# Set-up and first tile of a fused convolution and two-layer MLP kernel on one core: put-off low parts, an earlier split, PE work during the convolution, paired remainders

## The reference, cut to what matters

```python
out = np.einsum('hk,bskhg->bshg', softmax(weight), x_unfolded)   # convolution
h = x @ w_in1;  g = h / (1 + exp(-1.702 h));  x2 = g @ w_out1    # layer 1
h = x2 @ w_in2
P = a0 + a1*h + a2*h**2 + a3*h**3
Q = 1 + |b0|*|h| + |b1|*h**2
out = (P / (Q + 1e-6)) @ w_out2                                  # layer 2
```

## Time and profile before

| | |
|---|---|
| Median of three runs | 1391.59 us (1391.28 to 1391.95) |
| The profiled execution: its own time | 1396.26 us |
| The profiled execution: span in the trace | 1394.1 us |
| PE busy | 1324.5 us, 95% of the span, 4800 instructions |
| DVE, ACT, POOL busy | 1107.4 (79%), 979.4 (70%), 326.0 (23%) us |
| First matmul of step n = 0 | 25.33 us into the span |
| DMA | 20.37 MB, 15 GB/s on the mean |

### The profile page before, as it was taken

The page is one execution under the profiler, slowest core; times in us unless marked ns, Lnnn a source line. Parts: engine busy times, 40 slices in busy tenths (PEclk is TensorE's granted clock), DMA queues, the critical chain, the costliest instruction groups (busy, mean ns, idle before and its releaser), DMA issues. The chain is left out here.

```text
span 1394.1 us, 14800 instructions
## 1 busy us (share of the span) xinstructions
PE 1324.5 (95%) x4800; PEld 699.2 (50%) x4800; DVE 1107.4 (79%) x1204; ACT 979.4 (70%) x1161; POOL 326.0 (23%) x150
## 2 busy tenths in 40 slices
PE   2999999999999999999999999999999999999876
PEld 1445555555555555555555555555555555545332
DVE  5228888888888888888888888888888888877885
ACT  4237767777776777777777777777777777776774
POOL 3202222222222222222222222222222222222222
PEclk9999999999999999999999999999999999999998
DMA  8100000000000000000000000000000000000000
GB/s 207 38 12 0 11 1 23 1 12 12 1 23 0 23 0 11 11 0 23 0 23 0 11 11 0 23 0 23 0 11 12 1 12 1 12 0 12 0 12 11
DMA packets 32883, 20.37 MB, mean 15 GB/s; under 512 B 10321, under 2 KB 30801, under 8 KB 32849
## 3 DMA queue, kind: packets, MB, share of 16 engines
q1 hardware_dynamic: 32372, 19.93, 5.2%
q10 hardware_dynamic: 477, 0.01, 0.0%
HBM read 13.64 MB, written 6.29 MB: 14 GB/s over the span
## 5 line engine op out<-in xcount | busy, mean ns | idle before, releaser
L675 POOL TENSOR_TENSOR work<-work 128x1024 f32<-128x1024 f32 x128 | 303.6, 2372 | 1006.1 <-ACT work L430 1003.1
L271 PE MATMUL acc_a<-g,down 128*128 128x512 f32 x1024 | 477.9, 608 | 0.0
L271 PEld LDWEIGHTS acc_a<-g,down 128*128 128x128 f32 x1024 | 183.6, 190 | 293.5 <-issue 293.5
L571 DVE TENSOR_TENSOR work<-work,h 128x1024 f32<-128x1024 f32 x128 | 156.4, 1222 | 187.8 <-ACT work L430 187.6
L277 PE MATMUL acc_b<-g,down 128*64 128x512 f32 x1024 | 272.6, 608 | 31.1 <-DVE x_a_lo L589 16.0
L426 ACT ACTIVATE work<-h,par 128x1024 f32<-128x1024 f32 x128 | 142.8, 1116 | 182.3 <-PE h L265 181.6
L257 PE MATMUL h<-x_a_hi,up_a_hi 128*128 128x512 f32 x512 | 234.7, 458 | 25.5 <-DVE x_b L561 16.8
L456 ACT ACTIVATE work<-work 128x1024 f32<-128x1024 f32 x128 | 136.2, 1064 | 154.8 <-POOL work L675 152.9
L258 PE MATMUL h<-x_a_lo,up_a_hi 128*128 128x512 f32 x512 | 201.8, 394 | 0.0
L259 PE MATMUL h<-x_a_hi,up_a_lo 128*128 128x512 f32 x512 | 201.2, 393 | 0.0
L260 PE MATMUL h<-x_b,up_b_hi 128*128 128x512 f32 x512 | 200.6, 392 | 0.0
(11 more groups left out here) (75 smaller groups left out, 979.3 us busy)
## 6 DMA issues: line engine op xcount, KB each, us to landing
out<-y_out SPq DMA_DIRECT2D x16, 384.0 KB, 2.5
x_in_a<-in_x SPq DMA_DIRECT2D x16, 256.0 KB, 2.8
down<-in_moe_w_out SPq DMA_DIRECT2D x8, 384.0 KB, 6.1
x_in_b<-in_x SPq DMA_DIRECT2D x32, 64.0 KB, 2.5
work<-in_moe_w_in SPq DMA_DIRECT2D x8, 256.0 KB, 6.3
work<-in_moe_w_in SPq DMA_DIRECT2D x16, 128.0 KB, 6.6
wts<-in_weight ACTq DMA_DIRECT2D x2, 0.4 KB
wts<-in_weight SPq DMA_DIRECT2D x2, 1.3 KB
```

The lines of the kernel that those rows point to most:

```text
L271: last = mm(l.acc_a[:], l.down[:, f, 0:P], l.g[:, slot, k, :], start=f == 0, stop=f == STEPS - 1)
L571: tt(tu, tu, h, ALU.mult).then_inc(t2_ready, 1)
L675: tt(m, sq[(s - LAG_RATIO) % 2], seed, ALU.mult).then_inc(m_ready, 1)
```

## The change

It touches set-up and tile 0 alone. Six things are done:

1. POOL's `weights_lo(L1, c)` for c = 1 to 3 wait until DVE's split of tile 0 is done (x1_lo_done 3); chunk 0 is done by DVE, between its convolution and its split.
2. ACT's `split_x1(0, 0)` stands ahead of `weights_hi(L1, 2)`, after chunk 1.
3. The second half of x of tile 0 is transposed into a bank of `L1.h`, without a wait for ACT, and evacuated by DVE, not by ACT.
4. When 13 of the convolution's operations are done (WARM_AFTER), PE runs three float32 matmuls of 128x128 by 128x512 into `L1.acc_a`, whose result nothing reads.
5. In tile 0 `down_b` of the two units of a duo goes to the two halves of `acc_b`: unit k = 0 to rows 64 to 127, k = 1 to rows 0 to 63.
6. So at n = 8 the halves are added: ACT copies rows 0 to 63 into rows 64 to 127 of a new tile `x2_part`, DVE adds `acc_b`'s rows 64 to 127 to it, and the split of the remainder reads the sum.

```diff
+WARM_AFTER = 13
...
+            def down_b_apart(l, d, slot, k):
+
+                row = l.acc_row if k == 0 else DB - l.acc_row
+                return mm(acc_b[row:row + DB, :], l.down[:, 2 * d + k, P:D], l.g[:, slot, k, :],
+                          start=d == 0, stop=d == DUOS - 1)
...
+                    bank = L1.h[:, 0, :] if isinstance(tile, int) and tile == 0 else turned
...
-                    if live(v1):
+                    if isinstance(v1, int) and 0 <= v1 < DUOS:
+                        down_b_apart(L1, e1, (s - LAG_DOWN1) % 2, k)
+                    elif live(v1):
                         down_b(L1, e1, (s - LAG_DOWN1) % 2, k)
...
             pe.wait_ge(ident_ready, 1)
             transpose_x(0, 0)
-            pe.wait_ge(x_evacuated, 1)
             transpose_x(0, 1)
+            pe.wait_ge(x_evacuated, 2)
+            pe.wait_ge(conv_steps, WARM_AFTER)
+            for _ in range(3):
+                mm(L1.acc_a[:], ident[:], xt_a[:, HALO:], start=True, stop=True)
...
-                    fn(L2.x_b[DB:P, 1 - p, :], acc_b[DB:P, :], ACT.Copy).then_inc(x2_hi_done, 1)
+                    if isinstance(t, int) and t == 0:
+                        fn(x2_part[DB:P, :], acc_b[0:DB, :], ACT.Copy).then_inc(x2_part_read, 1)
+                        act.wait_ge(x2_part_added, 1)
+                        fn(L2.x_b[DB:P, 1 - p, :], x2_part[DB:P, :], ACT.Copy).then_inc(x2_hi_done, 1)
+                    else:
+                        fn(L2.x_b[DB:P, 1 - p, :], acc_b[DB:P, :], ACT.Copy).then_inc(x2_hi_done, 1)
...
             evacuate_x(0, 0)
-            evacuate_x(0, 1)
             weights_hi(L1, 0, stage1, w1_hi)
             act.wait_ge(abs_ready, 1)
             fn(root[:, 1:2], root[:, 0:1], ACT.Sqrt).then_inc(setup_act, 1)
             weights_hi(L1, 1, stage1, w1_hi)
+            split_x1(0, 0)
             weights_hi(L1, 2, stage1, w1_hi)
-            split_x1(0, 0)
             weights_hi(L1, 3, stage1, w1_hi)
...
+                    whole = acc_b
+                    if isinstance(t, int) and t == 0:
+                        whole = x2_part
+                        dve.wait_ge(x2_part_read, 1)
+                        tt(x2_part[DB:P, :], acc_b[DB:P, :], x2_part[DB:P, :], ALU.add).then_inc(x2_part_added, 1)
...
+            dve.wait_ge(x_transposed, 2)
+            nc.vector.tensor_copy(xt_b[:, HALO:], L1.h[:, 0, 0:HALF]).then_inc(x_evacuated, 1)
             dve.wait_ge(setup_act, 2)
...
             for op in conv_ops(0):
                 op().then_inc(conv_steps, 1)
+            first = slice(0, CW)
+            dve.wait_ge(w1_hi, 1)
+            tt(L1.up_a_lo[:, first], stage_a[:, first], L1.up_a_hi[:, first].bitcast(F32), ALU.subtract)\
+                .then_inc(w1_lo, 1)
+            tt(up_b_lo[0:DB, first], stage_b[0:DB, first], L1.up_b_hi[0:DB, first].bitcast(F32), ALU.subtract)\
+                .then_inc(w1_lo, 1)
             split_x1(0, 0)
...
-            for c in range(CHUNKS):
+            pool.wait_ge(x1_lo_done, 3)
+            for c in range(1, CHUNKS):
                 weights_lo(L1, c, w1_hi, w1_lo)
```

More of the change, by code:

```diff
@@ L141, in build_program @@
         y_b = sb("y_b", [P, HALF])
+        x2_part = sb("x2_part", [P, NT])
         y_out = sb("y_out", [P, BLOCKS, D])
@@ L158, in build_program @@
         h1_ready = sem("h1_ready"); g1_ready = sem("g1_ready"); g1_used = sem("g1_used")
+        x2_part_read = sem("x2_part_read"); x2_part_added = sem("x2_part_added")
         x2_hi_done = sem("x2_hi_done"); x2_lo_done = sem("x2_lo_done")
@@ L285, in transpose_x @@
                 else:
+                    bank = L1.h[:, 0, :] if isinstance(tile, int) and tile == 0 else turned
                     for j in range(BLOCKS // 2):
-                        last = nc.tensor.transpose(turned[:, j * P:(j + 1) * P],
+                        last = nc.tensor.transpose(bank[:, j * P:(j + 1) * P],
                                                    x_in_b[:, j, :, :].rearrange("p h d -> p (h d)"), ident[:])
@@ L575, in step @@
                 if s == S_X2 and tile_live(t):
+                    whole = acc_b
[3 more added lines that the diff above has]
+                        tt(x2_part[DB:P, :], acc_b[DB:P, :], x2_part[DB:P, :], ALU.add).then_inc(x2_part_added, 1)
                     dve.wait_ge(x2_hi_done, 2 * t + 1)
-                    tt(L2.x_b[0:DB, 1 - p, :], acc_b[DB:P, :], L2.x_b[DB:P, 1 - p, :].bitcast(F32), ALU.subtract)\
+                    tt(L2.x_b[0:DB, 1 - p, :], whole[DB:P, :], L2.x_b[DB:P, 1 - p, :].bitcast(F32), ALU.subtract)\
                         .then_inc(x2_lo_done, 1)
```

## The result

The changed kernel takes 1380.80 us, median of five runs (1377.76 to 1383.67), against 1391.95 (1391.28 to 1393.62): a ratio of 0.991, 95% interval 0.989 to 0.993. It is faster by 11.2 us; forecast were 17.3 and 1374.3 us, with a range to 1381.5. The profiled execution took 1380.80 us, 15.5 less than the profiled one of before, with a span of 1378.8.

What follows compares the result with a forecast made beforehand. PE, 95% busy, was taken as the bound, with DVE's chain ahead of its start and a low clock in its first steps. Gains 12.2 + 6.1 - 1.0 = 17.3 us gave 1374.3 us, 8-in-10 range 1372.5 to 1381.5.

Steps and rivals of the forecast that it cites:

- Evacuation: In tile 0's set-up, evacuation by DVE lets the convolution start at 8.55, not 9.01: gain 0.45 us.
- POOL put off: In tile 0's set-up, the convolution takes 7.77 us, not 13.81, with POOL at rest: gain 6.04 us.
- The extra row: Three matmuls during tile 0's convolution start at 13.2, last 5.1 to 5.4 us, delay nothing and likelier than not raise the clock.
- Side by side: In tile 0, a duo's two remainders in separate halves take about 1.0 us, saving 0.87; seven further downs give 6.1 us.
- The joining: At n = 8, 1.38 us is added to a chain with slack 0.37, so PE waits 1.0 us, once.
- the step from 22.4 to 29.8: PE's early steps, clock up: GELU from 23.2, step 1 from 24.3 to 27.0, down product to 29.8; gain so far 12.2 us.
- ACT's queue: In set-up, chunk 3 comes about 20.6 to 21.3; rounding (1.14) and table load (1.28) put the first GELU at 23.0 to 23.7.
- the base of the sum: Whole kernel: 17.3 us off the profiled 1396.26, itself 4.67 over the median, gives 1379.0 profiled and 1374.3 against the median.
- the 10.9 us of fp32r steps ahead of the first brought none: In PE's first steps before the change, 10.9 us of fp32r work brought no clock rise; both rises came inside unbroken float32 rows.
- rival 3: In tile 0, the shorter remainder keeps the clock low: steps about 10.4 us, not 5.4; with all seven 1414; chance 0.03.
- Rival 1: The clock rises not in the extra matmuls but in duo 0's down product: gain 12.5, 1379.1 us; chance 0.30.
- Rival 4: PE's start is held by another wait, such as ACT's table load: 1 to 3 us less gain, 1375 to 1377; chance 0.08.

## Why the prediction was right or wrong

**Right, by its own steps.**
- DVE was the chain ahead of step 0, by the reading of its last row above. Evacuation: start of the convolution 8.46 (forecast 8.55). POOL put off: 7.76 us (7.77). The two subtractions cost 1.21, not 1.45. PE's start came at 19.34 (19.7), and the gain of it was 6.0 us, not 5.6.
- The extra row began at 13.27 (13.2), took 5.27 (5.1 to 5.4), delayed nothing, and the clock was up when step 0 began, in each of the eight traces that have a row ahead of it. That the rise falls within the row did not always hold: without the pairs and with POOL beside the convolution its six rows took 5.46, the low clock's pace to the end, and the rise came behind it.
- Side by side: four acc_b rows in 1.01 us (30.22 - 29.21), saving 0.85 (0.87), and the four weight loads of both halves went in together, within 0.20 us. The rule that the prediction cites from the Trainium skill (TensorE: Matmul & The Clock Gate, "The mechanism") does not hold here: both halves use all rows, and the loads overlap all the same. The joining: a wait of 1.05 (1.0). Seven downs less the wait, 7 x 0.85 - 1.05 = 4.9, is what the middle shows.

**Wrong: the step from 22.4 to 29.8**, "the GELU from 23.2 ... lets step 1 go at 24.3, and it is through at 27.0". Two terms failed in it.
- ACT's queue was priced a little low: chunk 3 came at 21.39 and the GELU at 23.86; step 1 at 24.93, 0.6 late.
- The idle time of PE, 1.9 us by my own numbers, was priced at nothing for the clock, because the only fall in the rows came with 4.53. It was 2.84 (2.51 in the second trace), and the clock fell: step 1 took 4.28 us (24.93 to 29.21), not 2.7. That is 1.6. Filling the time, or shortening it to 1.11, kept the clock up: both experiments show it in their traces, and the granted clock of all their runs agrees.

So step 2 started at 32.39, not 30.2 (29.8 and the transposes): 2.2 of the 17.3 were missed. With 0.25 less from the middle and 0.5 more from the tail, the forecast was about 2.0 too high, and 17.3 - 2.0 is the 15.3 between the two spans (15.5 between the two times).

**Wrong: the base of the sum.** Between the forecast gain of 17.3 and the measured 11.2 lie 6.1 us, of which 1.8 are the difference to the 15.5 of the profiles. The other 4.3 us are not in the changed kernel. I worked the gain out from the profiled execution of before, 4.67 over the median, and took it off the median whole. The second trace of before shows what such a difference is made of: 2.7 us of it was the place of the rise. A low-clock stretch that was longer than usual was counted as if every run had it. The median of before minus what is constant (1389.3 of span, less 1334.15 and 17.5) puts its usual step 2 at about 37.7, by an estimate; from there to 32.4 there are 5.3 us to win, not 10.

**Luck in the range.** 1380.8 lies inside 1372.5 to 1381.5, but no case that the range was made of is what happened: one had the clock up and kept, the other had it low until duo 0's down product. The upper end was also close: the second median of the changed kernel, 1381.8, and five of its eleven runs with it, lie above 1381.5.

**Wrong: "the 10.9 us of fp32r steps ahead of the first brought none"**, and rival 3, which took only the unbroken float32 rows to bring the rise. In the second trace of before, in both versions without the row and in the one with only the early split the clock rose during or between fp32r steps, with no float32 row ahead. Rival 3 never showed: all traces have step 2 at the high clock. Rival 1 in its pure form, no rise before step 0, is in no trace of the changed kernel, yet its time (1379.1) is nearer to the result than the forecast: the clock was won and lost again. Rival 4 named the right instruction, ACT's table load, but as holding PE's start, which was not held; the load held step 1, and its price did not include the clock.

**The extra row** did what it was to do and was worth nothing: a step 0 that is 2 us shorter only waits longer for ACT, and behind this longer wait the clock was lost in nine of eleven runs, by their granted clock, against one of five without the row.

## What to carry to other kernels

When work is added to keep PE's clock up, look at the next wait of PE behind it as well: here 2.8 us behind one short step undid it, and moving one rounding behind the first GELU gave 3 to 4 us more with the row, but only 0.4 without it. Take gains in a stretch whose clock varies from at least two traces, or from the execution that stands at the median, before subtracting them from a median. A constant middle (here the same to 0.4 us among all traces with pairs, and to 0.1 among those without) makes such a kernel readable: cut the span where the variation ends.

## What the runs showed of the hardware that was not expected

- The clock fell after much shorter idle times than the tail's 4.53: 2.84, 2.51 and, without the pairs, 2.86; in the version with POOL beside the convolution it fell about 1.4 us into step 0 after an idle time of 2.03. In the traces of the versions with the GELU first, waits of up to 1.62 left it up. In all four of these falls PE was at work again: the granted clock still reads 1.00 up to the start of the work, and drops 0.1 to 1.4 us into it.
- The place of the rise moved by 6 us between two executions of the same kernel (about 40.7 and 34.8), with the same work at the same times; this alone made 2.7 us between their times. After PE's start the rise came some 15 us later in the first of them and 9 in the second, but only some 3 in the version with the early split alone, whose step 0 is the same work.
- The granted clock in the windows reads 1.00 all through the first low stretch of a trace (25.3 to 40.7 in the kernel before), although matmuls there take 0.63 us and not 0.39. In this stretch only their durations tell the level.
- The landing of chunk 3 moved by 0.56 us between two traces (21.39 in the changed kernel, 21.95 in the version with the idle time filled), which the first GELU followed one to one.
